# A 3008-point transform cut by its prime factors 64 and 47, its 47-point stages as four small products on quarters of the array

## The reference

```python
X = np.fft.rfft(x, axis=1)                      # x: (2, 3008, 256)
Y = X * (filt_r + 1j * filt_i)[None, :, :]      # 1505 frequencies
y = np.fft.irfft(Y, n=3008, axis=1)             # as 6016 tokens
h = y @ w_in;  z = np.maximum(0.01 * h, h) @ w_out         # 256 -> 2048 -> 256
h = z @ w2_in; r = np.maximum(h, 0.0); out = (r * r) @ w2_out
```

## Time and profile before

| what | us |
|---|---|
| median of 3 runs (1085.27 to 1086.64) | 1085.84 |
| the profiled execution | 1085.68 |
| its span, first to last instruction | 1083.9 |
| filter: first instruction to the first product of the layers | 114.27 |
| the units' loop: last turn ahead of it to the last inverse's end | 69.1 |

### The profile page before, as it was taken

How to read it: one execution, slowest core, us unless ns; L and a number is a source line. 1 busy time by engine, 2 the same in 40 slices (tenths; PEclk the granted TensorE clock), 3 DMA queues, 4 the chain that set the end, 5 groups by cost and what they waited for, 6 DMA issues and landing times.

```text
span 1083.9 us, 14070 instructions
## 1 busy us (share of the span) xinstructions
PE 1079.8 (100%) x5104; PEld 914.2 (84%) x5104; DVE 772.2 (71%) x1184; ACT 567.0 (52%) x983; POOL 295.9 (27%) x286
## 2 busy tenths in 40 slices
PE   9999999999999999999999999999999999999998
PEld 9888888888888888888899888888888888888998
DVE  2996889777677677676666776776766766766676
ACT  3555665555465465555454554554554554554544
POOL 0789334324324324224220220220120120120000
PEclk9999999999999999999999999999999999999999
DMA  9878400012112112112244200000100100100100
GB/s 324 235 231 262 136 1 1 23 44 59 44 44 59 44 44 58 44 44 55 56 158 160 72 1 1 40 1 1 40 1 1 40 1 1 39 1 1 40 1 34
DMA packets 70053, 66.09 MB, mean 61 GB/s; under 512 B 40800, under 2 KB 55648, under 8 KB 69984
## 3 DMA queue, kind: packets, MB, share of 16 engines
q1 hardware_dynamic: 69696, 64.90, 19.4%
q10 hardware_dynamic: 288, 0.30, 0.1%
HBM read 41.19 MB, written 23.99 MB: 60 GB/s over the span
## 4 chain that ended last, share of the span: by engine, by line
PE 100%; ACT 0%; issue 0%; POOL 0%; POOLq 0%
PE PS L966 16%; PE PS L968 16%; PE PS L967 16%; PE PS L974 14%; PE PS L976 14%; PE PS L975 14%; PE PS L907 3%; PE PS L917 3%; PE PS L880 2%; PE PS L935 2%; PE PS L896 1%; PE PS L870 0%; ACT YT L704 0%; POOL WARM L337 0%; POOLq L1189 0%
## 5 line engine op out<-in xcount | busy, mean ns | idle before, releaser
L646 ACT ACTIVATE GH<-GF 128x512 fp32r<-128x512 f32 (+1 forms) x384 | 238.8, 622 | 224.3 <-DVE GF L821 116.5
L827 DVE TENSOR_TENSOR GL<-GF,GH 128x512 fp32r<-128x512 f32 (+1 forms) x384 | 258.8, 681 | 104.9 <-ACT GH L646 99.3
L966 PE MATMUL PS<-GH,WOH 128*128 128x512 f32 (+1 forms) x768 | 296.2, 386 | 0.0
L968 PE MATMUL PS<-GH,WOL 128*128 128x512 f32 (+1 forms) x768 | 296.1, 386 | 0.0
L967 PE MATMUL PS<-GL,WOH 128*128 128x512 f32 (+1 forms) x768 | 296.1, 386 | 0.0
L974 PE MATMUL PS<-XH,WIH 128*128 128x512 f32 (+1 forms) x672 | 259.8, 387 | 0.0
L976 PE MATMUL PS<-XH,WIL 128*128 128x512 f32 (+1 forms) x672 | 259.1, 386 | 0.0
L795 DVE TENSOR_TENSOR GF<-PS,GF 128x512 f32<-128x512 f32 (+1 forms) x96 | 65.3, 680 | 164.0 <-ACT GF L617 163.9
L968 PEld LDWEIGHTS PS<-GH,WOL 128*128 128x128 f32 x768 | 144.2, 188 | 26.9
L967 PEld LDWEIGHTS PS<-GL,WOH 128*128 128x128 f32 x768 | 144.3, 188 | 26.7
L966 PEld LDWEIGHTS PS<-GH,WOH 128*128 128x128 f32 x768 | 144.2, 188 | 26.7
(11 more groups left out here) (76 smaller groups left out, 959.0 us busy)
## 6 DMA issues: line engine op xcount, KB each, us to landing
zu<-U SPq DMA_DIRECT2D x32, 192.0 KB, 2.9
V<-zu SPq DMA_DIRECT2D x12, 512.0 KB, 4.9
FL<-in_filt SPq DMA_DIRECT2D x16, 336.0 KB, 4.6
out_y<-YT SPq DMA_DIRECT2D x5, 1024.0 KB, 4.3
X<-in_x SPq DMA_DIRECT2D x8, 512.0 KB, 8.8
wi<-PWH SPq DMA_DIRECT2D x16, 224.0 KB, 2.5
wi<-PWL SPq DMA_DIRECT2D x16, 224.0 KB, 3.1
WIH<-wi SPq DMA_DIRECT2D x8, 448.0 KB, 3.5
```

The costliest lines, as they stand in the source:

```text
L646: nc.scalar.activation(GH[:, g, 0:width(s)], GF[:, g, 0:width(s)], ACT.Copy).then_inc(g_hi[kind], 1)
L827: nc.vector.tensor_tensor(GL[:, g, 0:w], GF[:, g, 0:w], GH[:, g, 0:w].bitcast(f32), ALU.subtract).then_inc(g_lo[kind], 1)
L966: nc.tensor.matmul(acc, wh, xh, start=first, stop=False)
L968: return nc.tensor.matmul(acc, wl, xh, start=False, stop=last)
```

## The change

The transform is cut by the prime factors instead: with 64 and 47 coprime, and the tokens taken in the order (47 n1 + 47-residue times 64) modulo 3008, no twiddle factors are needed, and one 47-point table serves all j. The n2 of a token and of 47 minus it are folded (sums and differences) by the signs in the table of the 64-point stage, so the 47-point stages have 48 rows for sums and differences each. They stand at partitions 0 to 47 and 64 to 111. A unit is now four j of one half (UJ = 4): 2 x 8 = 16 units. `spectrum` and `inverse` are four products each, of 48 rows, 64 columns of weights and 512 columns of data, each on another quarter (64x64) of TensorE's array; the first of a half's eight units has two of them cut in two for j = 0. All weights are in one small tile (TW, 112x384), and the signs in another (SG); the tables TB and their loads are gone. The filter's product is complex with a real and an imaginary part side by side: DVE makes one product of 112x1024 and two of 112x512 for a unit, POOL a difference and a sum of 112x512. TensorE's order is spectrum(i+2), turn(i+3), inverse(i). `turn` writes one bank for each of the two arrays and has those two alone, `inverse` two banks alone; the spectrum has two sets of two. Forming the first layer's weights moves out of the loop: three of the eight blocks ahead of it (their loads among those of x, their rounding on DVE), the rest behind it. Of the 24 sequences, three stand ahead of inverse(14), three ahead of inverse(15), fourteen behind the loop, and the last four among the first products of the layers, as before.

The diff, cut to its core:

```diff
+UJ = 4
+NU = NJ // UJ
+UNITS = 2 * NU
...
+FSLOTS = 6
+RINGS = 3
...
+    AF = [at(f"AF{r}", [KR, 2, B, 2 * 128], f32, (24 + 4 * r) * KB) for r in range(RINGS)]
+    BF = [at(f"BF{r}", [KR, 2, B, 2 * 128], f32, (o_wi + 49 * KB, 0, 4 * KB)[r]) for r in range(RINGS)]
...
+    DM = at("DM", [128, 3, 128], f32, o_s + 2 * KB)
+    TW = at("TW", [KR, 6, IM], f32, o_s + 2 * KB + 1792)
+    SG = at("SG", [KR, NU, 2], f32, o_s + 2 * KB + 2 * 1792)
...
+            for b in range(B):
+                for g in range(len(XG)):
+                    load_x(b, g)
+                    if (b, g) in X_THEN_W:
+                        load_w1i(X_THEN_W.index((b, g)))
...
+                if i in (2, 4, 6):
+                    load_w1i(WI_EARLY + (i - 2) // 2)
+                if i == NU + 1:
+                    for n in range(NU - RINGS, NU):
+                        sp.wait_ge(*stored(n))
+                if 0 <= i - NU - 1 < MH // 4:
+                    load_v(0, i - NU - 1, 1, 0, NJ)
+            sp.wait_ge(p_ps, 4 * UNITS)
+            load_w1o(0)
+            for n in range(UNITS - 1 - RINGS, UNITS - 1):
+                sp.wait_ge(*stored(n))
+            load_v(1, 0, 2, 0, NJ - UJ)
+            sp.wait_ge(*stored(UNITS - 1))
+            load_v(1, 0, 2, NJ - UJ, NJ)
+            for g in range(2, MH // 4):
+                load_v(1, g, 1, 0, NJ)
...
+            for i in range(UNITS):
+                a, c = AF[i % RINGS], BF[i % RINGS]
+                pool.wait_ge(prod, 3 * i + 3)
+                nc.gpsimd.tensor_tensor(a[:, 0], a[:, 0], c[:, 1], ALU.subtract).then_inc(yf_sb, 1)
+                nc.gpsimd.tensor_tensor(a[:, 1], a[:, 1], c[:, 0], ALU.add).then_inc(yf_sb, 1)
...
-                act.wait_ge(s2_ps, i + 1)
-                nc.scalar.activation(S2[:, i % 2, :, :, :].rearrange("p b j d -> p (b j d)"), PS[0:K2, (i + 1) % 2, :], ACT.Copy).then_inc(s2_sb, 1)
+                for b in range(B):
+                    act.wait_ge(s2_ps, 2 * i + b + 1)
+                    nc.scalar.activation(S2[:, i % 2, b, :, :].rearrange("p j d -> p (j d)"), PS[0:KR, b, :], ACT.Copy).then_inc(s2_sb, 1)
             def back(i):
-                act.wait_ge(u_ps, i + 1)
-                if i >= USLOTS:
-                    n = i - USLOTS
-                    act.wait_ge(z_out[n // PAIRS][n % USLOTS], 16 * (n % PAIRS // USLOTS + 1))
-                nc.scalar.activation(U[:, i % USLOTS, :, :].rearrange("p k e -> p (k e)"), PS[0:K2, 4 + i % 2, :], ACT.Copy).then_inc(u_sb, 1)
+                act.wait_ge(u_ps, 4 * i + 4)
+                if i >= RINGS:
+                    act.wait_ge(z_out[i % RINGS], 32 * (i // RINGS))
+                for js in range(2):
+                    nc.scalar.activation(U[:, i % RINGS, 2 * js:2 * js + 2, :].rearrange("p j e -> p (j e)"), PS[0:KR, 6 + js, :], ACT.Copy).then_inc(u_sb, 1)
...
-                P = PS[0:KR, 2 + i % 2, :].rearrange("p (b d) -> p b d", b=B)
...
-                nc.vector.tensor_tensor(YF[:, i % 3, :, :], P, fr.to_broadcast([KR, B, 2 * 128]), ALU.mult).then_inc(prod, 1)
...
-                nc.vector.scalar_tensor_tensor(XF[0:R, i % 3, :, :], P[IM:KR], -1.0, fi.to_broadcast([R, B, 2 * 128]),
-                                               ALU.mult, ALU.mult).then_inc(prod, 1)
...
-                nc.vector.tensor_tensor(XF[IM:KR, i % 3, :, :], P[0:R], fi.to_broadcast([R, B, 2 * 128]),
-                                        ALU.mult).then_inc(prod, 1)
+                    dve.wait_ge(sg_in, 16)
+                if i >= RINGS:
+                    dve.wait_ge(yf_sb, 2 * (i - RINGS + 1))
+                    dve.wait_ge(u_ps, 4 * (i - RINGS + 1))
+                P = PS[0:KR, 2 + 2 * (i % 2):4 + 2 * (i % 2), :].rearrange("p c (b e) -> p (c b) e", b=B)
+                fr, fi = FL[:, f, 0:1, :], FL[:, f, 1:2, :]
+                a, c = (t[r].rearrange("p c b e -> p (c b) e") for t in (AF, BF))
+                nc.vector.tensor_tensor(a, P, fr.to_broadcast([KR, 2 * B, 2 * 128]), ALU.mult).then_inc(prod, 1)
+                for k in range(2):
+                    d = slice(128 * k, 128 * k + 128)
+                    nc.vector.scalar_tensor_tensor(c[:, :, d], P[:, :, d], SG[:, u, k:k + 1], fi[:, :, d].to_broadcast([KR, 2 * B, 128]),
+                                                   ALU.mult, ALU.mult).then_inc(prod, 1)
...
-                half, j = i // PAIRS, 2 * (i % PAIRS)
-                if i >= 2:
-                    pe.wait_ge(s2_sb, i - 1)
+                half, u = i // NU, i % NU
+                if i == 0:
+                    pe.wait_ge(n1_pad, 2)
+                    pe.wait_ge(dft_rest, 16)
+                    pe.wait_ge(n1_sb[0], CH)
+                if i == NU:
+                    pe.wait_ge(n1_sb[1], CH - 2)
+                    pe.wait_ge(n1_late, 2)
                 for b in range(B):
-                    for k in range(2):
-                        mm = nc.tensor.transpose(PS[0:K2, (i + 1) % 2, 256 * b + 128 * k:256 * b + 128 * k + 128],
-                                                 TT1[half][:, b, j + k, :], DM[:, 2, :])
-                mm.then_inc(s2_ps, 1)
+                    if i >= 1:
+                        pe.wait_ge(s2_sb, 2 * i - 1 + b)
+                    for k in range(UJ):
+                        q = 2 * (UJ * u + k)
+                        mm = nc.tensor.transpose(PS[0:KR, b, 128 * k:128 * k + 128],
+                                                 TT1[half][:, b, q:q + 2, :].rearrange("p q r -> p (q r)")[:, 0:KR], DM[:, 2, :])
+                    mm.then_inc(s2_ps, 1)
             def spectrum(i):
-                pe.wait_ge(s2_sb, i + 1)
-                pe.wait_ge(tb_in[i % PAIRS], 16)
+                pe.wait_ge(s2_sb, 2 * i + 2)
+                if i == 0:
+                    pe.wait_ge(tw_in, 16)
                 if i >= 2:
                     pe.wait_ge(prod, 3 * (i - 1))
-                for k in range(2):
-                    mm = nc.tensor.matmul(PS[0:KR, 2 + i % 2, :].rearrange("p (b k d) -> p b k d", b=B, k=2)[:, :, k, :], TB[0:K2, i % PAIRS, k, 0:KR],
-                                          S2[:, i % 2, :, k, :], start=True, stop=True)
-                mm.then_inc(p_ps, 1)
+                for part in range(2):
+                    rows = slice(IM * part, IM * part + R)
+                    for js in range(2):
+                        o = PS[IM * js:IM * js + IM, 2 + 2 * (i % 2) + part, :].rearrange("p (b k d) -> p b k d", b=B, k=2)
+                        y = S2[rows, i % 2, :, 2 * js:2 * js + 2, :]
+                        if i % NU == 0 and js == 0:
+                            nc.tensor.matmul(o[:, :, 0], TW[rows, 1, :], y[:, :, 0], start=True, stop=True)
+                            mm = nc.tensor.matmul(o[:, :, 1], TW[rows, 0, :], y[:, :, 1], start=True, stop=True)
+                        else:
+                            mm = nc.tensor.matmul(o, TW[rows, 0, :], y, start=True, stop=True)
+                        mm.then_inc(p_ps, 1)
             def inverse(i):
-                pe.wait_ge(yf_sb, i + 1)
-                if i >= 2:
-                    pe.wait_ge(u_sb, i - 1)
-                for k in range(2):
-                    mm = nc.tensor.matmul(PS[0:K2, 4 + i % 2, 256 * k:256 * k + 256].rearrange("p (b d) -> p b d", b=B),
-                                          TB[:, i % PAIRS, k, KR:], YF[:, i % 3, :, 128 * k:128 * k + 128], start=True, stop=True)
-                mm.then_inc(u_ps, 1)
+                pe.wait_ge(yf_sb, 2 * i + 2)
+                if i >= 1:
+                    pe.wait_ge(u_sb, 2 * i)
+                else:
+                    pe.wait_ge(n1_sb[1], CH - 2)
+                    pe.wait_ge(n1_late, 2)
+                for js in range(2):
+                    rows = slice(IM * js, IM * js + R)
+                    for part in range(2):
+                        o = PS[IM * part:IM * part + IM, 6 + js, :].rearrange("p (k b d) -> p k b d", k=2, b=B)
+                        y = AF[i % RINGS][rows, part, :, :].rearrange("p b (k d) -> p k b d", k=2)
+                        if i % NU == 0 and js == 0:
+                            nc.tensor.matmul(o[:, 0], TW[rows, 4 + part, :], y[:, 0], start=True, stop=True)
+                            mm = nc.tensor.matmul(o[:, 1], TW[rows, 2 + part, :], y[:, 1], start=True, stop=True)
+                        else:
+                            mm = nc.tensor.matmul(o, TW[rows, 2 + part, :], y, start=True, stop=True)
+                        mm.then_inc(u_ps, 1)
...
-                if i + 3 == PAIRS:
-                    pe.wait_ge(n1_sb[1], CH - 2)
-                    pe.wait_ge(n1_late, 2)
+                if i + 2 < UNITS:
+                    spectrum(i + 2)
                 if i + 3 < UNITS:
                     turn(i + 3)
-                if i + 2 < UNITS:
-                    spectrum(i + 2)
-                if i >= UNITS - DRAIN:
-                    sequence(i - UNITS + DRAIN)
+                if i >= UNITS - 2:
+                    for c in drained(i):
```

(3 more changed lines are left out.)

## The result

The changed kernel takes 1078.38 us (median of 4 runs, 1077.3 to 1078.81), the kernel before 1085.77 beside it; the ratio is 0.993, with a 95% interval of 0.9912 to 0.9947. It is 7.4 us faster, where 22.8 were forecast (1063): the direction was right, the size three times too large. The profiled execution took 1077.3 us with a span of 1075.2.

The account below looks back on a forecast made before the run. TensorE was taken to bound the whole span, DVE and POOL little under it. The layers were to start at 77.3 + 14.6 = 91.9, 22.4 us earlier: 1085.68 less 22.4, forecast 1063 us, range 1057 to 1097.

Parts of the forecast that it names:

- The quarters side by side, unit 2.93: Loop on TensorE: transposes 0.88, two steps of 0.86 with four quarters at once, mode changes 0.33; 2.93 us a unit.
- the forecast's low end for a step: Spectrum or inverse in the loop: 0.86 us if the four quarters run side by side, 3.46 if one behind the other.
- All three rivals: Loop on TensorE: passes in program order (0.21, 1098 us), weight loads one at a time (0.14, 1077), no overlap (0.07, 1144).
- the first rival: Loop on TensorE: passes start in program order, each behind the one before; unit 5.10, time 1098 us; chance 0.21.
- the second rival: Loop on TensorE: weights load one pass at a time, step 1.3, unit 3.8, time 1077 us; chance 0.14.
- DVE 2.69 and POOL 2.55: Filter products in the loop: 2.69 us a unit on DVE and 2.55 on POOL, both under TensorE's 2.93.
- The seam, 14.6: From last inverse to layers: six chunks, a wait of 2.1 for V, eight chunks in 7.1; 14.6 us, before 15.2.
- The loop's start, 32.5: Ahead of the loop: first spectrum ends at 26.94, then DVE, POOL and a handover; inverse(0) starts at 32.5 us.
- x ends near 20.5 ... cost nothing, 1 if late: Loads ahead of the loop: three weight loads add 2.0 us, x ends near 20.5, wanted at 22.4; no cost, 1 if late.
- The six sequence chunks ... cost nothing: End of the loop: chunks ahead of the last two inverses, 2.7 us each time, fill places lacking spectrum and transposes; cost nothing.
- POOL's weight work ... keeps ahead: Behind the loop: three weight blocks of about 4.3 us on POOL stay ahead, as each serves 10 us of layer products.

Follow-up runs that it names:

- e11: Changed kernel, but each quarter's product waits until the one before it in its step has ended: 1275.76 us.
- e2: Changed kernel with V's second half loaded in six even loads of 512 KB, all behind the last store: 1074.93 us.
- e8: Changed kernel with V's second half loaded behind the last store, its first two groups in one 1 MB load of 128 partitions: 1078.34 us.
- e4: Changed kernel with 25 small products on zeros filling TensorE's wait for V: 1079.37 us.
- e1: Changed kernel with only one of three early weight loads left between the x loads, one behind x, one in the loop: 1077.80 us.
- e7: e2 with the first six filter loads held until the last but one load of x has landed: 1074.18 us.
- e5: e2 with one chunk of sequence products ahead of each of the last two inverses, the other four behind: 1073.02 us.
- e6: e2 with weight chunk 6's split and rounding and chunk 7's sums and rounding moved one step earlier: 1075.12 us.
- e9: e2 with BF's third buffer moved, all late weight work ahead of the layers, and one sequence chunk ahead of the last inverses: 1075.66 us.
- e13: Changed kernel with e2's loads, e10's filter, e9's buffer place, one sequence chunk ahead of the last inverses, one weight chunk within the layers: 1070.94 us.
- e14: e13 plus 2 and 3 small products ahead of the first stage's last chunks and 8 in the wait for V: 1071.64 us.
- e10: e2 with e5's edit and the filter laid out with 128 rows instead of 112: 1073.26 us.

## Why the prediction was wrong

- **The quarters side by side, unit 2.93: right.** 2.90 was measured. A spectrum right behind an inverse takes 0.86, as by the forecast's low end for a step; transposes behind quarters and quarters behind transposes take 1.02, so each change between whole array and quarters costs some 0.15 (forecast 0.163). That agrees with the Trainium skill, page "TensorEngine Tiling (Array Packing)", section "Tiling Modes", by which such a change drains TensorE. The Trainium skill, page "TensorE: Matmul & The Clock Gate", section "Part 3: Packing small matmuls — row/col tiling", gives 3.07 times for four tiles by rows; here four quarters gave 3.46 / 0.86, 4.0 times, or 3.4 with the change of mode in it, where 3.46 is the forecast's estimate for passes one behind the other. All three rivals fall: no step takes two or four passes' time, and eight weight loads fit under a step. The strict program order on which the first rival rests does not hold here, as L961 ahead of L959 shows. The measured time lies next to the second rival's 1077, but by chance: its sign, a unit near 3.8, is absent. e11 shows that without the overlap there is no gain.
- **DVE 2.69 and POOL 2.55: right.** 1.225 + 2 x 0.742 = 2.71 by the means, and 1.277 + 1.280 (L444) = 2.56.
- **The seam, 14.6: this step failed most.** The prediction had V's small part land about 7.5 us behind the last inverse, at 340 to 390 GB/s; it was 12.0: the store landed at 4.7 (forecast 4.2), V 7.24 behind it (forecast 3.3). Those rates belong to loads of 128 partitions; with the new loads of 112 and 16 it was 221 to 242 (e2, e8). The wait of 2.1 became 6.6, and the clock, taken as constant, fell in it: 2.0 to 2.3 us more (e4). The two, 4.5 and 2.3, are the 6.8.
- **The loop's start, 32.5: too early by 3.0.** "x ends near 20.5 ... cost nothing, 1 if late" was wrong: x landed at 23.6. The prediction took the fall of the rate near 18.5 for the end of x, but before, the last load of x goes out at 8.4 and lands 12.9 us later, at 21.3:

```profile
L214 SPq DMA_DIRECT2D X<-in_x x16: 387/440/692, 0.7 to 8.4; - x16
...
DMA to landing us min/median/max: 3.0/7.7/12.9
```

  The 2.4 from there to 23.6 are near the 2.0 that the prediction gave the weights (1.6 by e1); the filter loads beside the end of x were not the reason (e7). So the data cost 1.6 at turn(0). The other 1.4 is not the data: POOL is done with the first product at 34.0, but TensorE has a spectrum and eight transposes ahead of the inverse in its order, until 35.5.
- **"The six sequence chunks ... cost nothing": wrong.** Three chunks take 2.88 us where spectrum and transposes took 1.9, so the last inverse came 1.4 later than the late start explains; with one chunk each it came 2.8 sooner (e5).
- **"POOL's weight work ... keeps ahead": wrong, up to 2.4 us.** It kept ahead of the products that need it, but DVE beside it was slower, which the prediction did not ask. e6, e9, e13 and e14 show the loss going with the work; 0.9 us of it are waits of TensorE for a slowed split. That the slowing needs both engines on SBUF at once is not shown.
- **Open:** what makes x land anywhere from 22.6 to 27.2 us; e7 and e10 removed two suspects without an effect on it. Open too: the 1.5 us of the layers that stand in no wait.

## What to carry to other kernels

A forecast of a faster loop is half done when the loop is right: the same data still have to come in and go out, and everything that had been hidden behind the longer loop (here a store and a load in a row, weight work on another engine, weights among the inputs) has to be timed again against the shorter one. Load with all 128 partitions and in even pieces; a load cut to start early may come later for it. A shortfall of TensorE's work can cost twice, as waiting and as a slower clock after it.

## What the runs showed that was not expected

- Loads of fewer than 128 partitions: 221 to 247 GB/s with 112 (V, with a load of 16 behind it, and filter) against 372 to 412 with 128, at the same busy share of the DMA engines, about 1.0.
- Products on one quarter at a time, each waiting for the one before, left the granted clock at 0.50 from 46.9 to 268.8 us of e11, with TensorE busy 98% of a stretch in it; four at a time kept it at 1.00 with TensorE busy 100%.
- DVE's splits took 1.7 us each instead of 0.6 beside an unbroken run of GpSimd's work, and GpSimd's own instruction (L407) 1.75, where 1.29 stands before.
- The clock's fall at the seam: 0.79 in 90 to 92 us after an idle stretch that began at 87.1, then 0.50; in e2, after an idle stretch half as long, the same. It fell after 2.05 us of idleness in e5 and 1.88 in e10 (the 64 products 9.04 us), and not after 1.95 in e9 and 1.38 in e13 (7.41).
